# Attention stage of a fused kernel: per-head score matmuls in two row groups, three probability buffers, a new order of transposes, weight rounding on VectorE

## The reference

```
B, H, S, D = 4, 8, 576, 64          # float32
scores = (q @ k.T) / sqrt(D)
mask_local   = (rel >= 0) & (rel < 32)                    # heads 0..3, rel = query - key
mask_strided = (rel >= 0) & (query % 32 == key % 32)      # heads 4..7
scores = where(mask, scores, -1e9); scores -= max(scores)
attn = exp(scores); attn /= sum(attn) + 1e-9
out  = attn @ v                                            # [B, H, S, D]
x = out, heads side by side: [B * S, H * D] = [2304, 512]
```

## Time and profile before

| what | value |
|---|---|
| median of 3 runs | 608.15 us (606.93 to 610.79) |
| the profiled execution | 607.21 us, its span 605.4 us |
| TensorE (PE) busy | 580.0 us, 96% |
| VectorE (DVE) busy | 314.1 us, 52% |
| ScalarE (ACT) busy | 232.5 us, 38% |
| GpSimd (POOL) busy | 144.5 us, 24% |
| attention stage | from the start to about 132 us |

### The profile page before, as it was taken

How to read it: one execution, slowest core, us unless ns; L and a number is a source line. 1 busy time by engine, 2 the same in 40 slices (tenths; PEclk the granted TensorE clock), 3 DMA queues, 4 the chain that set the end, 5 groups by cost and what they waited for, 6 DMA issues and landing times.

```text
span 605.4 us, 11066 instructions
## 1 busy us (share of the span) xinstructions
PE 580.0 (96%) x3555; PEld 469.8 (78%) x3556; DVE 314.1 (52%) x746; ACT 232.5 (38%) x725; POOL 144.5 (24%) x154
## 2 busy tenths in 40 slices
PE   4999999998999999999999999998999999899995
PEld 3676776776888788888888878987989973398894
DVE  5899999956566666665566623258212111130210
ACT  3788888852333333433343332212112221121120
POOL 5555555552100111224322300110000111101001
PEclk9999999999999999999999999999999999999999
DMA  8966777300000062000000000000960105400000
GB/s 175 196 161 158 168 170 170 93 10 19 17 17 17 24 237 90 18 17 35 17 17 17 35 1 18 33 35 1 374 231 17 50 18 195 163 7 33 15 17 35
DMA packets 68875, 47.21 MB, mean 78 GB/s; under 512 B 54744, under 2 KB 56760, under 8 KB 68848
## 3 DMA queue, kind: packets, MB, share of 16 engines
q1 hardware_dynamic: 66928, 41.08, 24.0%
q0 software_dynamic: 1920, 5.77, 2.6%
HBM read 37.40 MB, written 9.96 MB: 78 GB/s over the span
## 4 chain that ended last, share of the span: by engine, by line
PE 76%; issue 8%; POOL 7%; DVE 3%; DMA 2%; SPq 2%; ACT 1%; POOLq 0%; DVEq 0%; ACTq 0%
PE pair L990 17%; PE bank L592 16%; PE pair L592 16%; PE bank L1005 15%; POOL work L564 4%; PE pair L1098 3%; POOL w_lo L571 3%; PE pair L1675 2%; PE bank L1118 1%; DMA out<-xT,s_idx 1%; PE pair L1658 1%; SPq L435 1%; DMA arena<-in_k 1%; PE pair L1130 1%; PE pair L713 1%
## 5 line engine op out<-in xcount | busy, mean ns | idle before, releaser
L990 PE MATMUL pair<-x_hi,lead_hi 128*128 128x256 f32 x288 | 82.0, 285 | 0.0
L990 PE MATMUL pair<-x_lo,lead_hi 128*128 128x256 f32 x288 | 81.5, 283 | 0.0
L990 PE MATMUL pair<-x_hi,lead_lo 128*128 128x256 f32 x288 | 81.5, 283 | 0.0
L784 ACT ACTIVATE work<-pair,neg_max 96x128 f32<-96x128 f32 (+2 forms) x176 | 61.6, 366 | 18.6 <-PE bank L724 15.0
L1566 POOL TENSOR_TENSOR rstd<-ln_small 128x1 f32 (+1 forms) x18 | 26.4, 1467 | 171.4 <-DVE ln_small L659 171.4
L1061 POOL DMA_INDIRECT out<-work,lead_sidx x18 | 17.9, 992 | 199.6 <-ACT work L1045 168.4
L592 PE MATMUL pair<-w_hi,x_hi 128*128 128x512 f32 x144 | 58.5, 406 | 0.2 <-ACT arena L773 0.2
L564 POOL TENSOR_TENSOR work<-work,row_inv 96x512 f32<-96x512 f32 (+3 forms) x48 | 44.7, 932 | 54.5 <-DVE row_inv L872 54.5
L592 PE MATMUL bank<-w_hi,lnT_hi 128*128 128x512 f32 x144 | 56.3, 391 | 1.1 <-DVE lnT_lo L1292 1.1
L592 PE MATMUL pair<-w_hi,x_lo 128*128 128x512 f32 x144 | 56.5, 392 | 0.0
L990 PEld LDWEIGHTS pair<-x_hi,lead_hi 128*128 128x128 f32 x288 | 55.2, 192 | 1.3 <-issue 0.8
(11 more groups left out here) (234 smaller groups left out, 1178.7 us busy)
## 6 DMA issues: line engine op xcount, KB each, us to landing
entry<-in_moe_w SPq DMA_DIRECT2D x12, 1024.0 KB, 10.2
arena<-in_q SPq DMA_DIRECT2D x32, 144.0 KB, 2.9
arena<-in_k SPq DMA_DIRECT2D x32, 144.0 KB, 3.4
x_dram<-work SPq DMA_DIRECT2D x18, 256.0 KB, 2.0
arena<-in_moe_w SPq DMA_DIRECT2D x8, 512.0 KB, 7.5
arena<-in_v SPq DMA_DIRECT2D x16, 144.0 KB, 2.6
work<-in_v SPq DMA_DIRECT2D x16, 135.0 KB
arena<-in_moe_w_in SPq DMA_DIRECT2D x8, 256.0 KB, 3.1
```

Of the source, the lines that this page charges most:

```text
L784: ins = act.activation(probs[g % 2][0:rows, cols], score_ps[g % 2][0:rows, cols], ACT.Exp, bias=neg_max[g % 2][0:rows, n:n + 1], accum_out ...
L990: ins = pe.matmul(lead_h_ps[n % 2][:, jj * BLK:(jj + 1) * BLK], a[:, w], b[:, x], start=(passes == 1), stop=(passes == 3 * KC))
```

## The change

- **Scores.** Keys are stored once. For each tile and head there is a matmul of its own, with 64 partitions of queries and keys, head 0 in the lower and head 1 in the upper ones. Head 0's scores go to the first bank of a pair and head 1's to the second; there is one mask matmul for each head, of half the columns. Both pairs, `pair0` and `pair1`, are used in turn.
- **Banks.** The output leaves `pair1`: turned probabilities have one bank and the output has one, where each had two.
- **Probabilities.** Three buffers in place of two; the third lies where `lnT_hi` is later. The sums and their inverses have three as well.
- **Order.** TensorE does turn_third(g+4) ahead of turn_probs(g-2); ScalarE does take_o(g-3) ahead of exps(g).
- **Weights.** `round_w` goes from ScalarE to the end of VectorE's groups 1 and 3.
- `take_k` copies both heads at once; of the zero fills of the keys only 32 columns are left.

```diff
+        with nc.sbuf_tensor("probs_third", [P, HALF], F32) as probs_third:
+            pass
         lnT_hi = sb("lnT_hi", FF, F32R)
...
-        row_sum = [sb(f"row_sum{b}", 4) for b in range(2)]
-        row_inv = [sb(f"row_inv{b}", 4) for b in range(2)]
+        row_stats = sb("row_stats", 6 * 4)
+        row_sum = [row_stats[:, b * 4:(b + 1) * 4] for b in range(3)]
+        row_inv = [row_stats[:, b * 4:(b + 1) * 4] for b in range(3, 6)]
...
-        k_T = [take(2 * (S + STRIDE)), take(2 * ST * SR)]
+        k_T = [take(S + STRIDE), take(ST * SR)]
         k_pad = [STRIDE, 0]
-        probs = [work[:, b * HALF:(b + 1) * HALF] for b in range(2)]
+        probs = [work[:, b * HALF:(b + 1) * HALF] for b in range(2)] + [probs_third[:, :]]
...
-        score_ps = [pair0[:, 0:HALF], pair0[:, HALF:2 * HALF]]
+        score_ps = [pair0, pair1]
...
-        pT_ps = [bank[0], bank[1]]
-        o_ps = [pair1[:, 0:HALF], pair1[:, HALF:2 * HALF]]
+        pT_ps, o_ps = bank[0], bank[1]
...
+        def score_cols(g, hh, n=0, count=1):
+
+            rows, keys = rows_keys(g)
+            return score_ps[g % 2][0:rows, hh * HALF + n * keys:hh * HALF + (n + count) * keys]
...
-                full = score_ps[g % 2][0:rows, 0:2 * len(tiles) * keys]
-                pe.matmul(full, ident_bf[0:rows, 0:rows], mask_of(g), start=True, stop=False)
+                for hh in range(2):
+                    pe.matmul(score_cols(g, hh, 0, len(tiles)), ident_bf[0:rows, 0:rows], mask_of(g), start=True, stop=False)
                 for n, t in enumerate(tiles):
-                    ins = pe.matmul(score_ps[g % 2][0:rows, n * 2 * keys:(n + 1) * 2 * keys],
-                                    q_cols(local, t), k_cols(local, t), start=False, stop=(t == tiles[-1]))
+                    for hh in range(2):
+                        part = slice(hh * D, (hh + 1) * D)
+                        ins = pe.matmul(score_cols(g, hh, n), q_cols(local, t)[part], k_cols(local, t)[part],
+                                        start=False, stop=(t == tiles[-1]))
                 ins.then_inc(scored, 1)
...
                 pe.wait_ge(normed, c + 1)
-                wait(pe, p_out, c - 1)
+                wait(pe, p_out, c)
...
                 pe.wait_ge(p_out, c + 1)
-                wait(pe, o_out, c - 1)
+                wait(pe, o_out, c)
...
+                    if next_third(i, g):
+                        turn_third(*next_third(i, g))
                     if lagged(i, g, 2):
                         turn_probs(*lagged(i, g, 2))
-                    if next_third(i, g):
-                        turn_third(*next_third(i, g))
...
                 act.wait_ge(maxed, c + 1)
-                wait(act, p_turned, c - 1)
+                wait(act, p_turned, c - 2)
...
                 for g in range(NG):
+                    if lagged(i, g, 3):
+                        take_o(*lagged(i, g, 3))
                     if not (static(i) and i == NI):
                         exps(i, g)
                     if next_third(i, g):
                         take_q(*next_third(i, g))
-                    if lagged(i, g, 3):
-                        take_o(*lagged(i, g, 3))
...
-                    if g in (1, 3) and not (static(i) and i == NI):
-                        round_w(i, g // 2)
...
-            dve.memset(k_T[0], 0.0)
-            dve.memset(k_T[1], 0.0).then_inc(zeroed, 1)
+            dve.memset(k_T[0][:, 0:STRIDE], 0.0).then_inc(zeroed, 1)
...
-                heads = k_T[kind].rearrange("p (h n) -> p h n", h=2)
-                for hh in range(2):
-                    part = slice(hh * D, (hh + 1) * D)
-                    for dst, src in in_order(heads[part, hh, k_pad[kind]:], banks_of(n)[1][part], kind, m):
-                        ins = dve.tensor_copy(dst, src)
+                for dst, src in in_order(k_T[kind][:, k_pad[kind]:], banks_of(n)[1], kind, m):
+                    ins = dve.tensor_copy(dst, src)
...
+            def round_w(i, m):
+
+                if m == 0:
+                    dve.wait_ge(ld_w, 32 * (i + 1))
+                cols = bass.ds(i * HALF + m * KC * FF, HALF)
+                dve.tensor_copy(w_hi[:, cols], w_raw[:, cols]).then_inc(w_rounded, 1)
...
                         take_p(*lagged(i, g, 2))
                     if next_third(i, g):
                         take_k(*next_third(i, g))
+                    if g in (1, 3) and not (static(i) and i == NI):
+                        round_w(i, g // 2)
```

More of the change, by code:

```diff
@@ L359, in k_cols @@
         def k_cols(local, t):
-            kt = k_T[0 if local else 1].rearrange("p (h n) -> p h n", h=2)
+            kt = k_T[0 if local else 1]
             if local:
-                return kt[:, :, t * JR:t * JR + P]
-            return kt[:, :, t * SR:t * SR + NA * RES[t]]
+                return kt[:, t * JR:t * JR + P]
+            return kt[:, t * SR:t * SR + NA * RES[t]]
+        def score_cols(g, hh, n=0, count=1):
+            rows, keys = rows_keys(g)
+            return score_ps[g % 2][0:rows, hh * HALF + n * keys:hh * HALF + (n + count) * keys]
         def in_order(cols, ps, kind, m):
@@ L384, in mask_of @@
             rows, keys = rows_keys(g)
-            return m[0:rows, :].rearrange("p (n c) -> p n c", n=4)[:, 0:2 * len(tiles), 0:keys]
+            return m[0:rows, :].rearrange("p (n c) -> p n c", n=4)[:, 0:2 * len(tiles):2, 0:keys]
         def steps(eng, body, lag):
@@ L561, in normalise @@
                 n = 2 * len(tiles)
-                block = probs[g % 2][0:rows, 0:n * keys].rearrange("p (n c) -> p n c", n=n)
+                block = probs[g % 3][0:rows, 0:n * keys].rearrange("p (n c) -> p n c", n=n)
                 pool.wait_ge(inverted, NG * i + g + 1)
-                pool.tensor_tensor(block, block, row_inv[g % 2][0:rows, 0:n].unsqueeze(2).to_broadcast([rows, n, keys]),
+                pool.tensor_tensor(block, block, row_inv[g % 3][0:rows, 0:n].unsqueeze(2).to_broadcast([rows, n, keys]),
                                    ALU.mult).then_inc(normed, 1)
@@ L721, in turn_probs @@
                 pe.wait_ge(normed, c + 1)
-                wait(pe, p_out, c - 1)
+                wait(pe, p_out, c)
                 for n in range(2 * len(tiles)):
-                    ins = pe.transpose(pT_ps[g % 2][0:keys, n * rows:(n + 1) * rows],
-                                       probs[g % 2][0:rows, n * keys:(n + 1) * keys], ident[0:rows, 0:rows])
+                    ins = pe.transpose(pT_ps[0:keys, n * rows:(n + 1) * rows],
+                                       probs[g % 3][0:rows, n * keys:(n + 1) * keys], ident[0:rows, 0:rows])
                 ins.then_inc(p_turned, 1)
@@ L736, in values @@
                 pe.wait_ge(p_out, c + 1)
-                wait(pe, o_out, c - 1)
+                wait(pe, o_out, c)
                 for n, t in enumerate(tiles):
                     for hh in range(2):
-                        at_ = (2 * n + hh) * rows
-                        ins = pe.matmul(o_ps[g % 2][hh * D:(hh + 1) * D, n * rows:(n + 1) * rows],
+                        at_ = (hh * len(tiles) + n) * rows
+                        ins = pe.matmul(o_ps[hh * D:(hh + 1) * D, n * rows:(n + 1) * rows],
                                         v_tile(local, t, hh), probs_T[g % 2][0:keys, at_:at_ + rows],
@@ L780, in exps @@
                 act.wait_ge(maxed, c + 1)
-                wait(act, p_turned, c - 1)
[L782 to L786, removed]
+                wait(act, p_turned, c - 2)
+                for hh in range(2):
+                    for n in range(len(tiles)):
+                        at_ = hh * len(tiles) + n
+                        ins = act.activation(probs[g % 3][0:rows, at_ * keys:(at_ + 1) * keys], score_cols(g, hh, n),
+                                             ACT.Exp, bias=neg_max[g % 2][0:rows, at_:at_ + 1],
+                                             accum_out=row_sum[g % 3][0:rows, at_:at_ + 1])
                 ins.then_inc(exped, 1)
@@ L794, in take_o @@
                 nt = len(tiles)
-                src = o_ps[g % 2][:, 0:nt * rows]
+                src = o_ps[:, 0:nt * rows]
                 if local:
@@ L858, in maxima @@
                 dve.wait_ge(scored, c + 1)
-                dve.tensor_reduce(neg_max[g % 2][0:rows, 0:n],
-                                  score_ps[g % 2][0:rows, 0:n * keys].rearrange("p (n c) -> p n c", n=n),
+                heads = score_ps[g % 2][0:rows, :].rearrange("p (h m) -> p h m", h=2)[:, :, 0:n // 2 * keys]
+                dve.tensor_reduce(neg_max[g % 2][0:rows, 0:n].rearrange("p (h n) -> p h n", h=2),
+                                  heads.rearrange("p h (n c) -> p h n c", c=keys),
                                   AX.X, ALU.max, negate=True).then_inc(maxed, 1)
@@ L880, in take_p @@
                 dve.tensor_copy(probs_T[g % 2][0:keys, 0:2 * len(tiles) * rows],
-                                pT_ps[g % 2][0:keys, 0:2 * len(tiles) * rows]).then_inc(p_out, 1)
```

(1 more changed line is left out.)

9 lines of the change are left out of this document (2 added, 7 removed).

## The result

The changed kernel takes 622.24 us (617.72 to 623.74) beside 608.49 (606.93 to 610.79) for the one before, a ratio of 1.0194 with a 95% interval of 1.0156 to 1.0231. It is slower by 1.9%, and outside the forecast range. The profiled execution took 621.05 us, its span 619.3 us against 605.4.

A forecast was written before the change was run, and what follows sets the result against it. Three engines nearly in lockstep bound attention; then a loop through take_q: 13.2 + 0.48 delays + 0.93 wait = 14.6 us a round. Seven rounds at +0.25, less 1.1, gave 608.8; with full delays 613; forecast 610, range 598 to 616.

The forecast's parts named there:

- The granted clock is 1.00, the 2.4 GHz level, in both stretches: TensorE's clock, read from the kernel before in attention and behind it; no time was counted for a change of clock.
- The start doesn't gain: First round: TensorE waits for the first keys until 6.02 us anyway, so no gain there and only seven rounds count.
- the wait: VectorE's second weight rounding of a round, end of group 3, waits 0.93 us for GpSimd's subtraction; bounds 0 and 1.28.
- the bare loop: Attention: loop from mask g to mask g+2 through scores, maxima, exps, take_q and transposes, 13.2 us a round before VectorE's delays.
- I take half of the 0.95: VectorE's delays of maxima in groups 2 and 4, 0.95 us a round; half assumed hidden in another loop's slack, 0.48 counted.
- rival 1: VectorE's delays and wait come in full, rounding takes 0.65 us: 15.1 to 15.6 a round, 612 to 616 us; chance 0.18.
- the last round's -1.1: Last round of attention: input transposes gone from group 2 on, four groups save 0.3 us each, -1.1 us in all.
- rival 2: VectorE reaches the rounding before GpSimd's subtraction, no wait: 13.2 to 14.2 us a round, 600 to 607 us; chance 0.26.
- Row halves: Score matmuls in two row groups run at once: 0.3 us saved in a two-tile group, about 1.45 of TensorE's work a round.
- rival 4: Row halves don't overlap: 0.43 us more in the scores, 15.9 to 16.4 a round, 619 to 622 us; chance 0.07.
- VectorE's terms: VectorE in attention: take_k's copies halved, 0.35 us in a local third, 2.6 saved a round; each added weight rounding 0.40.
- Rival 3: The loop is estimated too long, TensorE sets the pace: 12.4 to 13.1 us a round, 593 to 599 us; chance 0.13.

The follow-up runs named there:

- e14: The changed kernel with three identity matmuls more ahead of each mask in the first round alone (the pad): 617.02 us, ratio 1.0106.
- e3: The changed kernel with VectorE's second weight rounding of a round in group 2 in place of group 3: 610.74 us, ratio 1.0003.
- e2: The changed kernel with TensorE's input transposes last in a group again, behind the probability transposes: 615.56 us, ratio 1.0109.
- e4: The kernel before with third probability buffer, new order and rounding on VectorE; scores, banks and key copies as before: 627.51 us, ratio 1.0285.
- e6: The kernel before with row groups, their single banks and the third buffer; old order, rounding on ScalarE: 624.08 us, ratio 1.0143.
- e9: e3 with two probability buffers in place of three: 643.84 us, ratio 1.0524.
- e8: e3 with twelve identity matmuls more on TensorE ahead of the first input transposes: 611.27 us, ratio 1.0030.
- e12: e10 with three identity matmuls more ahead of each mask in the first round alone: 605.62 us, ratio 0.9913.
- e13: The kernel before with the weight rounding on VectorE, in groups 1 and 2: 612.71 us, ratio 1.0037.
- e1: The changed kernel with the weight rounding back on ScalarE, at the end of its groups 1 and 3: 612.89 us, ratio 1.0047.
- e10: e3 with TensorE's old order, input transposes last in a group: 610.76 us, ratio 1.0017.
- e11: e3 with three identity matmuls more ahead of each mask in the first round alone: 608.27 us, ratio 0.9976.
- e5: The kernel before with only the weight rounding moved to VectorE, at the end of groups 1 and 3: 620.99 us, ratio 1.0204.

## Why the prediction was wrong

**The failed step** is the clock. "The granted clock is 1.00, the 2.4 GHz level, in both stretches" is true of the kernel before; the sum carries it over to the changed one without a term, and "The start doesn't gain ... So seven rounds count" puts the first round at nothing. I took TensorE's clock as a given, though the edit halves the score matmuls' columns in the part of the kernel where TensorE has the least to do. The first round, with its late rise, costs 4.8 us of span. The pad, which is work itself, brings 3.3 of them back in e14's trace; the ratios differ by 0.9%, 5.4 us, with wide intervals. The falls between cost 3.4. Of the 13.9 us over before up to 8.2 are this step's (the falls may have the wait as their cause, below). Without them 5.7 would be left, 614 us, inside the range. The 1.8 us behind attention are no more than what executions of one kernel differ by.

**The loop and its delays.** The 13.2 of the bare loop and the reasons for its delays fit what was measured: input transposes wait for `take_q`, 9.8 us in 29 places. The step "I take half of the 0.95" failed, mildly: the full sum was 15.1 and 15.00 was measured, so rival 1's pace was the true one. e3, which takes out the wait alone, has 13.95: 13.2 and 0.75 of the 0.95. Delays that I thought would hide in another loop's slack mostly did not. A slip stands beside it: seven full rounds of 15.1 and the last round's -1.1 give +3.9 and 612, where the sum says +5 (613); rival 2's 600 to 607 is in the same way 599 to 606.

**The wait** was right: 0.93 forecast, 0.96 measured (1.37 less 0.41), by the mechanism named. Not right was the premise of rival 2, that VectorE escapes if it comes ahead of the subtraction: in e2 it waits for the multiply before it as well. GpSimd's two operations stand one behind the other, so the obstacle is 2.3 us long, and there is no slack of 0.35.

**Row halves** overlap, so rival 4 fell: eight of them take 0.64 us from start to next phase (64.94 to 65.58), where 0.53 was counted and 0.96 is the sum without overlap. That the measured time lies near rival 4's 619 to 622 is chance, since its mechanism didn't come. The two-tile group saves 0.2 and not 0.3, so TensorE's own work falls by about 1.1 us a round (an estimate: five such groups at 0.16 to 0.24, nothing for the single tile) and not by 1.45. The worth of a round by e4, 1.4 to 1.8, is no confirmation of the 1.45, for it holds VectorE's spared copies as well.

**VectorE's terms** held: `take_k` 0.35 in a local third, the rounding 0.41 to 0.43 against 0.40.

**Rival 3** (12.4 to 13.1 a round) didn't come: no kernel here had a round under 13.6.

**Single banks** for output cost nothing with `take_o` in front, and up to 1.06 us at a time with it behind the exponentials (e6).

**The last round** gave 0.3 us back, not 1.1. By its last mask (136.10 against 124.62) it had given 0.9; its second rounding, at 133.62, lasts 2.17 us, and values behind it wait for VectorE.

**Open.** Falls of the clock in the middle of attention were seen in the profiled executions of the changed kernel, e2, e4 and e14, which have the long wait, and of e9; at the seam behind attention in e8, e12 and e13; in neither place in e1, e3, e6, e10 and e11, nor in e5, which has the wait. That stalls of TensorE bring them is likely, but one profiled execution each doesn't settle it. Nor is it shown why the late rise comes at 22 us in e3 and e9, 25 in e10 and 31 in the changed kernel, e1 and e2, with a like first round; chance may have a part in it. With the rise at 22 us, e3's second round starts at 26.74, only 1.2 behind before, so the 4.8 us needn't be in every execution. What the pad in rounds 2 to 7 would do wasn't tried.

## What to carry to other kernels

Where an edit makes TensorE's matmuls cheaper in a stretch in which it isn't the bound, ask what the granted clock will do: look for the first row at the upper level, and count what every later step of the chain costs at the lower one. Before work is moved to VectorE, list GpSimd's operations around the new place, and treat two of them back to back as one obstacle. Where several loops pass through one engine, don't halve its delays without a row that shows the slack: here 0.75 of 0.95 us came.

## What the runs showed of the hardware

- A VectorE operation between SBUF tiles that arrives during one GpSimd tensor operation doesn't get in ahead of the next: 1.90 us in e2, with 0.41 of its own. The Trainium skill, SBUF — State Buffer, "SBUF: two separate sides", says that the one that starts first has the shared pair for the whole instruction. Read as a lock that is free again at an instruction's end, the rounding would have begun at 69.55, and the trace disagrees: GpSimd's next operation, which the view has from 69.51 on, went first.
- TensorE's busy share doesn't tell the clock. In e14 its rows fill 10.00 of 10 us at a granted clock of 0.51; a row lasts longer at the lower level (0.90 us against 0.55), so full rows can be its effect. The Trainium skill, TensorE: Matmul & The Clock Gate, Part 1, says that the gate follows how busy TensorE has been recently; the padded first rounds agree (up at 14 or 15 us against 22 to 31).
- Executions of the kernel before go from 606.6 to 612.9 us, and the time goes with the mean granted clock: the four at 0.998 took 606.6 to 607.2 us, the nineteen at 0.988 took 611.1 to 612.9. Of the profiled executions, the one of before, e3's and e11's have no fall of the clock behind attention, a mean clock of 0.998 and 605.6 to 607.2 us. The others have one or two short ones (between 420 and 470 us, or 530 and 570), and e1's and e10's, where this is the only fall once the clock is up, have a mean of 0.995. Most of the spread of a kernel's times here is thus its clock.
- Mask to scores takes 0.31 us with two mask matmuls and row groups (64.63 to 64.94) where one mask of about as many columns took 0.21. The 0.1 us is the price of the second mask and of the change of form together; no run parts them.
